# Up products of two chained MLPs in Strassen's form, with weights loaded per step

## What is computed

```python
kv = einsum('bhsd,bhse->bhde', k, v)        # q, k, v: 4 x 8 heads x 576 x 64
out = einsum('bhsd,bhde->bhse', q, kv)
x = out / sqrt(mean(out * out) + 1e-06) * g_norm      # as 2304 tokens x 512
h = x @ w_in1                                # 512 x 2048
x = (h * sigmoid(1.702 * h)) @ w_out1        # 2048 x 512
h = x @ w_in2
y = (maximum(h, 0) + log1p(exp(-abs(h)))) @ w_out2
```

## Time and profile before

| | us |
|---|---|
| median of 3 runs | 849.14 |
| the profiled execution, its own time | 847.83 |
| its span, from first to last instruction | 846.0 |
| TensorE busy in the span | 832.7 |
| VectorE busy | 428.7 |
| ScalarE busy | 267.2 |
| GpSimd busy | 185.3 |

### The profile page before, as it was taken

The page is one execution under the profiler, slowest core; times in us unless marked ns, Lnnn a source line. Parts: engine busy times, 40 slices in busy tenths (PEclk is TensorE's granted clock), DMA queues, the critical chain, the costliest instruction groups (busy, mean ns, idle before and its releaser), DMA issues.

```text
span 846.0 us, 11740 instructions
## 1 busy us (share of the span) xinstructions
PE 832.7 (98%) x4296; PEld 702.6 (83%) x4296; DVE 428.7 (51%) x775; ACT 267.2 (32%) x505; POOL 185.3 (22%) x156
## 2 busy tenths in 40 slices
PE   7899999999999999999999999999999999999998
PEld 6787888998888888888888888888888888888897
DVE  4747434353334332444446754655565546555574
ACT  4664311111110211023234533433343333433343
POOL 0259400000000000004443532222212222222131
PEclk9999999999999999999999999999999999999999
DMA  9954300000000000003210100100010001000100
GB/s 308 348 195 154 120 26 1 1 2 0 1 1 1 0 0 0 0 0 100 98 51 25 50 1 1 50 0 0 0 50 0 0 0 50 0 0 0 50 2 26
DMA packets 13488, 36.13 MB, mean 43 GB/s; under 512 B 1553, under 2 KB 3217, under 8 KB 13457
## 3 DMA queue, kind: packets, MB, share of 16 engines
q1 hardware_dynamic: 12880, 35.39, 12.2%
q10 hardware_dynamic: 576, 0.33, 0.1%
HBM read 31.00 MB, written 4.72 MB: 42 GB/s over the span
## 4 chain that ended last, share of the span: by engine, by line
PE 93%; DMA 4%; DVE 1%; ACT 1%; issue 1%; DVEq 0%; ACTq 0%
PE ps L419 46%; PE ps L381 46%; DMA kv_in_sb<-k_v 4%; DMA tail_sb<-k_v 1%; PE ps L322 0%; DVE rms L591 0%; DVE xs L610 0%; PE ps L339 0%; DVE x_tok L603 0%; PE ps L360 0%; ACT sq_sb L464 0%; DVE gs L658 0%; PE ps L400 0%; ACT L555 0%; DVE xs L612 0%
## 5 line engine op out<-in xcount | busy, mean ns | idle before, releaser
L658 DVE CAST gs<-hid 128x512 fp32r<-128x512 f32 (+1 forms) x160 | 82.9, 518 | 275.7 <-PE ps L419 274.0
L381 PE MATMUL ps<-xs,w_shared 128*128 128x512 f32 (+1 forms) x960 | 210.1, 368 | 0.0
L381 PE MATMUL ps<-xs,w_own 128*128 128x512 f32 (+1 forms) x960 | 206.4, 368 | 0.1
L381 PEld LDWEIGHTS ps<-xs,w_shared 128*128 128x128 f32 x960 | 168.8, 188 | 30.6
L381 PEld LDWEIGHTS ps<-xs,w_own 128*128 128x128 f32 x960 | 167.8, 189 | 31.0 <-DVE xs L612 0.8
L294 POOL TENSOR_TENSOR stage<-stage 128x512 f32<-128x512 f32 (+1 forms) x80 | 94.5, 1182 | 290.6 <-DVE stage L640 290.6
L527 ACT ACTIVATE hid<-ps 128x512 f32<-128x512 f32 (+1 forms) x80 | 44.5, 557 | 262.1 <-PE ps L381 256.8
L660 DVE TENSOR_TENSOR gs<-hid,gs 128x512 fp32r<-128x512 f32 (+1 forms) x160 | 107.1, 670 | 5.6
L281 POOL TENSOR_TENSOR w_own<-stage,w_own 128x512 fp32r<-128x512 f32 x32 | 42.4, 1348 | 300.7 <-ACT w_own L457 300.6
L419 PE MATMUL ps<-gs,w_own 128*128 128x512 f32 (+1 forms) x480 | 105.2, 368 | 0.5 <-DVE gs L658 0.5
L531 ACT ACTIVATE stage<-ps 128x512 f32<-128x512 f32 (+1 forms) x80 | 44.5, 556 | 193.6 <-PE ps L381 175.4
(11 more groups left out here) (43 smaller groups left out, 390.9 us busy)
## 6 DMA issues: line engine op xcount, KB each, us to landing
stage<-moe_w SPq DMA_DIRECT2D x32, 512.0 KB, 3.3
kv_in_sb<-k_v SPq DMA_DIRECT2D x16, 512.0 KB, 9.6
q_sb<-q_t SPq DMA_DIRECT2D x16, 288.0 KB, 10.1
out<-xy SPq DMA_DIRECT2D x18, 256.0 KB, 2.2
tail_sb<-k_v SPq DMA_DIRECT2D x3, 256.0 KB, 11.2
tail_sb<-k_v ACTq DMA_DIRECT2D x1, 256.0 KB, 5.1
eye_sb<-eye ACTq DMA_DIRECT2D x1, 64.0 KB, 5.7
g_col<-g_norm ACTq DMA_DIRECT2D x2, 0.2 KB, 7.0
```

The lines of the kernel that those rows point to most:

```text
L381: mm = nc.tensor.matmul(bank, w[:, W_IN, wp, cols], xs[:, xp, k, 0:width], start=(k == 0 and (wp, xp) == (HI, HI)), stop=(k == KT - 1 and ...
L658: nc.vector.tensor_copy(gs[:, HI, s, at:at + width], g).then_inc(g_hi_made, 1)
```

## The change

Phase 0 and 1 now go over three chunks of 768 tokens, and in a chunk over 8 steps, each for a pair of d_ff tiles: 48 steps in all (`ALL`), 24 of each phase. The up product of a step is seen as a 2 x 2 by 2 x 2 block product: the halves of d_model (two tiles of 128 each), the two d_ff tiles, and the two halves of 384 tokens. Strassen's form (in Winograd's variant) makes it with seven block products in place of eight. Each block product is 6 matmuls of 384 columns (`product`, L514): two tiles of d_model by three. The other operand sums have to be made:

- Of the activations, once per chunk: `raw_x` on VectorE makes the four sums, `round_x` on ScalarE rounds all seven blocks, `low_x` on VectorE subtracts (768 columns each). 
- Of the weights, in every step: SyncE loads the four blocks of the pair (512 KB), GpSimd makes four sums (`w_sums`, 256 columns each), ScalarE rounds all seven blocks (`round_w_in`, 1792 columns), GpSimd subtracts (`w_low`, 1024 and 768 columns). The up weights no longer stay in SBUF, so this is done anew in each of the 48 steps; the down weights stay, and a pair is split in one instruction of 1024 columns (`w_out_low`), in steps 0 to 7 and 18 to 25.
- Of the results, in every step: ScalarE copies the first product out of PSUM (`first_product`), and five additions on VectorE (`add`) combine the banks with blocks in SBUF. Two banks, A and B, hold all products, so a product often waits until the one before it in its bank has been read.

The four result tiles of a step (C11, C21, C22, C12; 384 columns each) go through the activation. All but C11 are read from SBUF, not from PSUM. In phase 1 ScalarE makes the rounding copy (`round_g`) that VectorE made before. `down` of the step before is cut into pieces (`shares`) that are put between the seven products.

The core of the diff:

```diff
-    CHUNK = 512
-    FULL = T // CHUNK
-    DOWN_LAG = 3
+    HALF = 384
+    CHUNK = 2 * HALF
+    CHUNKS = T // CHUNK
+    ALL = 2 * CHUNKS * STEPS
+    PHASE1 = CHUNKS * STEPS
...
+            def w_sums(n):
+                w32 = w_in32[:, n % W_BUFS, LO]
+                pool.wait_ge(w_in_landed[n % W_BUFS], w_loads(n))
+                nc.gpsimd.tensor_tensor(w32[:, S3], w32[:, A11], w32[:, A21], ALU.subtract).then_inc(w_summed, 1)
...
+            for m in range(1, ALL + 1):
+                if m > PHASE1:
+                    softplus_fix(m - 1, C12)
+                if m == ALL:
+                    break
+                n = m + 2
+                if W_POOL <= n < ALL:
+                    w_sums(n)
+                if m >= PHASE1:
+                    softplus_fix(m, C11)
+                if W_POOL <= n < ALL:
+                    pool.wait_ge(w_hi_made, n - W_POOL + 1)
+                    w_low(n, slice(0, 4))
+                if w_out_of(m):
+                    w_out_low(m)
+                if m >= PHASE1:
+                    softplus_fix(m, C21)
+                if W_POOL <= n < ALL:
+                    w_low(n, slice(4, 7))
+                if m >= PHASE1:
+                    softplus_fix(m, C22)
...
+            def product(m, k):
+                bank = BANK_B if k in (P6, P7, P4) else BANK_A
+                new = k in (P1, P6, P5)
...
+                if k == P1:
+                    pe.wait_ge(w_split, 2 * m + 2)
+                    if m > 0:
+                        pe.wait_ge(added, ADDS * (m - 1) + C12_ADD + 1)
...
+                if k == P2:
+                    pe.wait_ge(t1_made, m + 1)
+                if k == P7:
+                    pe.wait_ge(added, ADDS * m + U2 + 1)
+                if k == P4:
+                    pe.wait_ge(added, ADDS * m + U3 + 1)
+                if k == P5:
+                    pe.wait_ge(hid_read, TILES * m + C11 + 1)
+                if k == P3:
+                    pe.wait_ge(added, ADDS * m + C22_ADD + 1)
...
+            def shares(m):
+                part = (0, 4, 6, 13, 14, 19, 24)
+                if m % STEPS == 0:
+                    part = (2, 4, 6, 14, 18, 24, 24)
...
+            for m in range(ALL):
+                came = 0
+                for k in range(PRODUCTS):
+                    product(m, k)
...
+                    if m > 0:
+                        down(m - 1, came, shares(m)[k])
+                        came = shares(m)[k]
...
+                if phase:
+                    back(m, C11)
+                    add(m, U3)
+                    softplus(m, C11)
...
+                if phase:
+                    low_g(m, C11)
+                add(m, C21_ADD)
...
+                add(m, C22_ADD)
...
+                if phase:
+                    back(m, C21)
+                    softplus(m, C21)
+                    low_g(m, C21)
+                else:
+                    gate(m, C21)
...
+                add(m, C12_ADD)
```

More of the change, by code:

```diff
@@ L17 @@
 HI, LO = 0, 1
-W_IN, W_OUT = 0, 1
 EPS = 1e-6
@@ L26, with build @@
 KV_BANK, RAW_EVEN, RAW_ODD, TURN_EVEN, TURN_ODD = 0, 1, 2, 4, 5
[L27 to L34, removed]
+BANK_A, BANK_B = 7, 0
+ACC_BANK, ACC_BANKS = 1, 6
+PRODUCTS = 7
+P1, P6, P2, P7, P4, P5, P3 = range(PRODUCTS)
+A11, A12, A22, S1, S2, S3, S4 = range(7)
+A21 = S1
+W_OF = (A11, S2, A12, S3, A22, S1, S4)
+B11, T2, B21, T3, T4, T1, B22 = range(7)
+U2, U3, C21_ADD, C22_ADD, C12_ADD = range(5)
+ADDS = 5
+C11, C21, C22, C12 = range(4)
+TILES = 4
+PLACE = ((0, 0), (1, 0), (1, 1), (0, 1))
+def build(nc, q_t, k_v, g_norm, w_in1, w_out1, w_in2, w_out2, eye, out):
     UNITS, _, S = q_t.shape
@@ new lines, in build, with w_out_of, tiles_done, wait_down @@
+        SWAP_FROM = PHASE1 - STEPS + 2
+        def w_out_of(m):
+            if m < STEPS:
+                return m, 0
+            if SWAP_FROM <= m < SWAP_FROM + STEPS:
+                return m - SWAP_FROM, 1
+            return None
+        def tiles_done(m):
+            return sum(KT if ci < CHUNKS else ACC_BANKS for ci in range(m // STEPS))
+        def wait_down(engine, m):
+            if m % STEPS == STEPS - 1:
+                engine.wait_ge(acc_tile_done, tiles_done(m + 1))
+            else:
+                engine.wait_ge(down_done, m + 1 - m // STEPS)
@@ L423, in chunk @@
-            def chunk(ci, width, phase, first=False, last=False):
-                n0 = ci * FT
-                for f in range(FT + DOWN_LAG):
-                    if first and f in (1, 2):
-                        turn(UNITS - 3 + f)
-                        pe.wait_ge(x_made, UNITS - 4 + f)
-                    if first and f == 3:
-                        pe.wait_ge(x_made, UNITS)
-                    if f < FT:
-                        up(f, n0, ci, width, phase)
-                    if f >= DOWN_LAG:
-                        down(f - DOWN_LAG, n0, ci, width, phase, last and f == FT + DOWN_LAG - 1)
@@ L445, in _ @@
+            down(ALL - 1, 0, down_size(ALL - 1))
         @block.scalar
         def _(act):
[L447 to L458 removed]
@@ new lines, in hidden @@
+            def hidden(m, tile):
+                i = TILES * m + tile
+                if tile == C11:
+                    act.wait_ge(prod_done, PRODUCTS * m + P2 + 1)
+                    h = ps[:, BANK_A, 0:HALF]
+                else:
+                    act.wait_ge(added, ADDS * m + (C21_ADD, C22_ADD, C12_ADD)[tile - 1] + 1)
+                    h = hid(m, tile)
+                if i >= 2:
+                    act.wait_ge(hid_read, i - 1)
+                if m < PHASE1:
+                    nc.scalar.activation(lg[:, i % 2], h, ACT.Sigmoid, scale=SIGMOID_SCALE).then_inc(log_made, 1)
+                else:
+                    i1 = i - TILES * PHASE1
+                    if i1 >= 2:
+                        act.wait_ge(fix_made, i1 - 1)
+                    nc.scalar.activation(ex[:, i % 2], h, ACT.Abs).then_inc(abs_made, 1)
+                    act.wait_ge(abs_made, i1 + 1)
+                    nc.scalar.activation(ex[:, i % 2], ex[:, i % 2], ACT.Exp, scale=-1.0).then_inc(exp_made, 1)
+                    act.wait_ge(exp_made, i1 + 1)
+                    nc.scalar.activation(lg[:, i % 2], ex[:, i % 2], ACT.Ln, bias=1.0).then_inc(log_made, 1)
```

740 lines of the change are left out of this document (440 added, 300 removed).

## The result

The changed kernel takes a median of 1022.77 us (4 runs, 1022.36 to 1023.23); the kernel before, run beside it, 848.91 (4 runs, 848.2 to 850.76). The ratio is 1.204, with a 95% interval of 1.202 to 1.207. The profiled execution has a span of 1021.3 us, 43.8 more than the 977.5 of the forecast's sum.

The account below looks back on a forecast made before the run. TensorE's columns bound the kernel before; VectorE's queue would bound phase 1 after. From 846.0 us, -45.0 + 2.5 + 127 - 7 + 13 + 11 + 17.5 + 8 + 4.5 gave a 977.5 span, about 980 us; forecast range 930 to 1030.

Parts of the forecast that it names:

- TensorE's columns: Up and down products on TensorE: 173.2 ns per 384-column matmul; up 45.0 us less, down 2.5 us more.
- The walk of phase 1: VectorE's queue followed through one phase 1 step: 20.7 us against TensorE's 15.4, adding 127 us, less 7 in the last steps.
- the 16.7 without any exclusion: Phase 1 step in us if VectorE and GpSimd never block each other: in-line chain plus the wait for Exp.
- the first rival: VectorE and GpSimd block each other less than read, phase 1 steps take 16.7 us: 866 us total; chance 0.17.
- Chunk boundaries: Sums, subtractions and copies of activations at five chunk changes: 11 us in phase 0, 17.5 in phase 1; bounds 10 and 45.
- the exclusion: VectorE instructions with two SBUF operands, or copies in SBUF, and GpSimd instructions run one after the other.
- Start: Step 0, with no down work to fill waits and GpSimd late with weights: 8 us more, bounds 5 and 15.
- Pair steps: The 13 phase 0 steps that also split a down pair: 1.0 us more each, 13 us; bounds 0 and 21.
- The end: C22 and C12 of the last step must be finished before down: 4.5 us more.
- TensorE as the bound: Rival: VectorE's chain fits under 15.4 us a step, so the kernel gets faster, 822 us; chance 0.10.
- The clock did fall: Rival: TensorE's stops bring 1.2 GHz, phase 1 steps take 30.8 us, total 1220 us; chance 0.05.
- The worse interlock: Rival: GpSimd holds up fix behind ScalarE's 1792-column rounding, boundaries cost the upper bound; 23 us a step, 1035 to 1080; chance 0.08.

Follow-up runs that it names:

- kernel 1: Changed kernel without loads, sums and subtractions for the up weights from step 26 on (old values used, ScalarE's 1792-column copy kept): 954.95 us.
- kernel 4: Changed kernel with C21 and C22 taken through VectorE by turns in phase 1 and some instructions reordered, none added or left out: 957.08 us.
- kernel 11: The interleaved order of kernel 4, without loads and GpSimd's work for the up weights from step 26 on: 904.07 us.
- kernel 7: Changed kernel with ScalarE rounding C11 before the next chunk's activation blocks in the last step of a phase 1 chunk: 1019.02 us.
- kernels 1 and 2: The second is the changed kernel with GpSimd's six weight instructions per step replaced by zero fills from step 26 on, loads kept: 954.11 us.
- kernel 6: Changed kernel with 16 extra matmuls (28 at boundaries) ahead of each first product in phase 1 to keep TensorE busy: 1026.02 us.
- kernel 3: Changed kernel with C12_ADD moved ahead of C21's whole activation in VectorE's queue in phase 1: 1104.88 us.
- kernels 8 and 9: Changed kernel with the down pair's split moved to the step's front, or behind the four weight sums: 1021.77 and 1040.78 us.

## Why the prediction was right, and where its sum was short

**TensorE's columns, right.** Between gaps six matmuls of 384 columns take 1.05 us (L514, then L553, phase 0):

```profile
234.91 1.20 PE L514 MATMUL ps<-xs,w_in 128*128 128x384 f32 x6
235.96 0.39 PE L553 MATMUL ps<-gs,w_out 128*128 128x512 f32 x1
```

from 234.91 to 235.96 it is 175 ns each, for the forecast's 173.2; an ordinary step of phase 0 takes 15.60, as forecast. Busy TensorE was to be about 790 us and is 868.1, 10% more. Matmuls at the half clock are part of that; the share was not worked out.

**The walk of phase 1, right.** Forecast 20.7, measured 20.36. Piece by piece, from one C12_ADD to the next (forecast, then the timeline): C22 3.54 and 3.40; C12 4.50 and 4.44; C11 5.31 and 5.33; the two additions 0.94 and 1.01; the wait for Exp 1.07 and 1.04; C21 4.90 and 4.67; C12_ADD 0.47 and 0.47. The 0.14 us that the blocked instruction saves, which the sum took from the earlier trace rows, is there again: the one at 701.30 ends 0.42 after GpSimd and not 0.56. So the literal reading of the Trainium skill (SBUF — State Buffer, "Who interferes with whom"), without this saving, was rightly left aside; but the 23.1 a step and the 58 us that the forecast gave for it don't follow from it. In a measured step six of VectorE's instructions are held, and six times 0.14 is 0.8 us, not 2.4. Nor do the 16.7 without any exclusion: the terms named for it, 13.3, 1.65 and 1.07, add up to 16.0. Neither number is in the forecast's sum; the 16.7 is in the 866 of the first rival. The runs show both causes by themselves. Without the work on weights the step loses 2.98 (kernel 1), in the better order 3.19 (kernel 4), with both 4.66 of the 4.9 above TensorE (kernel 11). The two alone add up to 6.2, more than the 4.9 that there are: below 15.4 TensorE is the bound.

**Chunk boundaries, the term that was mis-sized.** Forecast 11 and 17.5 us, 28.5 in all. Measured, as what the steps around a boundary take above their kind: 11.2 and 9.1 in phase 0, 11.5 between the phases, 14.8 twice in phase 1: 61 us. That is 33 of the missing 44, and the 61 lie above the forecast's upper bound of 45. The forecast let the work on activations fall into waits and left the exclusion out of it. Step 31, VectorE:

```profile
645.24 0.95 DVE L812 TENSOR_TENSOR xs<-xy,xs 128x768 fp32r<-128x768 f32 x1
646.11 3.15 DVE L801 TENSOR_TENSOR xs_f<-xy 128x768 f32<-128x768 f32 x1
649.36 0.96 DVE L801 TENSOR_TENSOR xs_f<-xs_f,xy 128x768 f32<-128x768 f32 x1
653.15 0.56 DVE L883 TENSOR_TENSOR gs<-gs_f,gs 128x384 fp32r<-128x384 f32 x1 [2.83 <-ACT gs L675]
```

and GpSimd and TensorE:

```profile
645.32 3.12 POOL L357 TENSOR_TENSOR w_in<-w_in_f,w_in 128x1024 fp32r<-128x1024 f32 x1 [0.67 <-ACT w_in L680]
...
655.57 2.29 PE L514 MATMUL ps<-xs,w_in 128*128 128x384 f32 x6 [5.74 <-DVE gs_f L848]
```

The sum of 0.95 us takes 3.15, behind the 1024-column split, which the subtraction at 645.24 had held up before (3.12 for 2.40). Then 2.83 us go on ScalarE's order (kernel 7). TensorE stops for 5.74. In step 7 two sums and a subtraction take 2.99, 3.15 and 2.37 us in a row. Without GpSimd's work on weights a phase 1 boundary costs 12.5 in place of 14.8 (kernel 1), or 10 in place of the 16.8 of kernel 4 (kernel 11). So GpSimd's work on weights makes 2 to 7 of it, by the order, and the greater part stays without it; it was not divided further between VectorE's own work and ScalarE's.

**Start, too low.** Forecast 8 with an upper bound of 15, measured about 22. By the forecast step 1 would begin at 52.15 + 1.9 (what the kernel before lost there, too, between its first up and its first down products) + 7.3 + 8 = 69.3; it begins at 82.04, and its first six matmuls take 2.26 at the half clock, another 1.1. The first up product starts at 56.00 and not at 52.15, since its operands must be split before; the copy of the first product (64.64) stands on ScalarE behind the last unit of the attention stage and 1.28 us of loading a table; and VectorE runs into GpSimd's splits of the third weights (69.62) and of the down pair (78.45, 2.38 for a cast of 0.36). The forecast walked step 0 as if it stood alone:

```profile
64.64 0.48 ACT L649 COPY gs_f<-ps 128x384 f32<-128x384 f32 x1
...
65.27 4.18 PE L514 MATMUL ps<-xs,w_in 128*128 128x384 f32 x12 [2.92 <-ACT gs_f L649]
...
67.00 4.24 POOL L357 TENSOR_TENSOR w_in<-w_in_f,w_in 128x1024 fp32r<-128x1024 f32 x2
...
69.62 2.04 DVE L861 TENSOR_TENSOR gs<-gs_f,gs 128x384 fp32r<-128x384 f32 x1
...
82.04 2.26 PE L514 MATMUL ps<-xs,w_in 128*128 128x384 f32 x6 [4.10 <-DVE gs_f L848]
```

The twelve matmuls at 65.27 run at the half clock, too (4.18 us). No experiment was made on the start: this division is read from the trace alone.

**Pair steps and the rest.** A phase 0 step with a pair costs 1.46 above 15.60, not 1.0: 19 us for 13, and step 1 another 1. The ordinary steps of phase 1 gave back 7 (22 times 0.34). The end is 2 shorter than the forecast, which counted both `down` and the drain in full. 33, 14, 7, -7 and -2 make 45, for 43.8 measured; the terms are rounded, and 1 us stays open. So the mechanism of the ordinary step was right and carried the largest term. That the total came out within 930 to 1030 owes something to luck: two terms lay outside their own bounds, both upwards, and 7 us more would have left that range.

**The rivals.** That the exclusion holds less than read (866 us) is out by the L879 and L848 rows and kernels 1 and 2. TensorE as the bound (822) would need a chain below 15.4; even kernel 11 has 15.70. The clock did fall, which got a chance of 0.05, but not as that rival said: it is 0.92 in the stretch 693 to 815 and 0.93 over the span, not at 1.2 GHz throughout. It fell after gaps of 2.39 to 2.85 us, shorter than the 3.6 that the forecast named, and kernel 6 shows that it cost ordinary steps nothing, since TensorE has the slack. At boundaries, at the start and in kernel 3 it may lie in the chain, and how much of those terms it makes stays open. The worse interlock (23 us a step, 1035 and more) did not come: the step is 20.36, and before each of its 96 `fix` GpSimd waits for `back` (L867), so none was late for ScalarE's rounding. But its other half did: boundaries cost more than the upper bound.

No version was faster than the kernel before. Against the 42.5 us that TensorE's columns save stand, in the best full version (span 955.3), 1.74 x 22 = 38 us of ordinary phase 1 steps, 71 at boundaries, 23 at the start and 19 in pair steps, read from its step lengths in the same way: 108.5 net, for 109.3 measured.

## What to carry to other kernels

Fewer matmuls pay only if the engine that makes their sums and reads their banks has the time: walk its queue in order, each round trip to another engine included, and boundaries and the start as carefully as the ordinary step. VectorE instructions with two operands in SBUF (and copies such as `back`) and GpSimd instructions that read SBUF take turns; in kernels 8 and 9 moving GpSimd's work within a step for the most part only moved the stall. Where a chain alternates between engines, two tiles side by side hide the round trips: here that was worth 66 us (1022.8 to 957.1) at the same instructions.

## What the runs showed of the hardware beyond the forecast

- A zero fill on GpSimd doesn't hold up a VectorE addition of two SBUF operands (0.56 us beside it), and takes 0.95 us for 1024 columns, where a subtraction takes 2.40.
- The granted clock fell to 0.92 with one gap of 2.39 to 2.85 us in each step of 20.36, with TensorE busy for 105.6 of 122 us; with the gap filled it was 1.00.
- GpSimd and VectorE take turns even where one has its instructions back to back (705.46, 705.58, 706.43, 706.92), and at long instructions both pay in one pair: 3.12 for 2.40 and 3.15 for 0.95.
